# Last GEMM of a fused attention and two-MLP kernel: seven products for both halves of K in two of its three units

## The chip, the cores and the metric

The kernel runs on one core of a Trainium2 chip. The time is that of the device in microseconds. Before the change it is 571.29 us, the median of three runs (570.75 to 573.59).

## The reference, cut to what matters

```
attn  = softmax(30 * tanh(q k^T / 8 / 30)) v          # 2 batches, 12 heads, 448 positions, 64 wide
x     = attn as 896 tokens x 768
x     = leaky(x @ w_in) @ w_out                       # 768 -> 2048 -> 768, slope 0.01
xn    = x / rms(x) * rms_g
out   = (silu(xn @ w_gate) * (xn @ w_val)) @ w_out2   # 768 -> 1536 -> 768
```

All in float32. The last line's second product is "the last GEMM": K = 1536, 768 output rows (the features; everything is held transposed), 896 columns (tokens).

## The kernel before, in words

Activations lie as 128 features by 448 tokens (S = 448), one such tile for each batch b, weights as 128 by 384 slabs (HALF). A float32 matrix is split into a high part (rounded to fp32r) and a low part (the rest), and a product is three matmuls: high weight by high activation, high by low, low by high. K is taken in 128-row steps (index c), three in a half of 384.

**Seven products.** A block of two row tiles by two batches is computed from seven half-size products instead of eight (Strassen's form as Winograd wrote it). P1, P5, P7, P6, P3, P2, P4 take, in this order, the activation operands B11, T1, T3, T2, B22, B21, T4. T1 to T4 are sums or differences of activation tiles; the weights of P5, P7, P6, P3 are sums too (`s_sum`, made by DVE in `s_part`). Each product is 9 matmuls (3 steps of K, 3 matmuls each). Its results are put together on DVE (`take_p5`, `take_p7`, `take_p6`, then the `value`, `gate` or `result` functions), and ACT keeps P1 in SBUF (`keep_p1`).

**Units.** The program counts units s. 8 to 19 are the twelve units of gate and value (seven products each, K = 768 whole), 20, 21, 22 the three units of the last GEMM (`UNITS` = 20, `LAST` = 23). In this text they are G12 for unit 19 and L1, L2, L3 for the last three. G12 makes the last two of 24 activation tiles (`weighted_1`, `weighted_0`, into `act_full`). In each of L1, L2, L3 the kernel before takes the first half of K (tiles 0 to 5) plainly, as eight half-size products (`plain`; weights PA, PB, PC, PD, 72 matmuls), and the second half (tiles 6 to 11) by the seven products (63 matmuls): 135 matmuls a unit. The operands are made once, before and in L1: plain splits by ACT and POOL during units 11 to 19, T1 to T4 and their splits around the joint of G12 and L1.

**Order.** It is written out by hand, engine by engine; every engine runs its list in order and waits on semaphores. A weight slab n goes through ACT (`weight_hi`: copy to the high part, once product n - 7 has freed the slot in a ring of seven), then POOL (`weight_lo`: raw less high), then PE. For four of seven the raw operand is an `s_sum` slot, which DVE may only rewrite when POOL has made the low part of the slab before in that slot. Raw weights come by DMA on SP's queue into four buffers, each loaded when POOL is done with the one before it there. Names and lines of before that the argument touches: `weight_hi` L648, `weight_lo` L538, `keep_p1` L656, `s_part` L972 to L981, `take_p5` L996, `take_p7` L1002, `take_p6` L1008, `z_t3` L1253, `z_t2` L1258, `z_t4` L1263, `z_lo` L1267, `z_hi` L835, the results L1274 to L1298, `product` L1509, `plain` L1686.

Of the kernel before, what the change touches and what calls it, by code (L numbers as in the profile page):

```python
# [17 lines left out]
def build(nc, qk, v, cap, w_in, w_out, w_gate, w_val, w_out2, rms_g, out, recips):  # L18
# [67 lines left out]

    with ExitStack() as ctx:
# [284 lines left out]
        def plain_hi(k, b):  # L372
            i = PLAIN.index((k, b))
            return plain_ring[:, cols(i)] if i < 8 else plain_spare[:, cols(i - 8)]

        def plain_lo(k, b):
            return act_lo[:, cols(2 * k + b)]

        def z_tile(blk, c):
            return {B22: act_tile(F0 + KH + c, 1), B21: act_tile(F0 + KH + c, 0), T3: act_tile(F0 + c, 1)}.get(blk, act_tile(F0 + c, 0))

        def t1(k, c):
            return k[:, cols(c)]

        def z_parts(*blks):
            return [(blk, c) for blk in blks for c in range(KH)]

        z_all = z_parts(B11, T3, T2, B22, B21, T4)  # L390
        z_count = {part: i + 1 for i, part in enumerate(z_all)}
# [1372 lines left out]
```

## Time and profile before

| | |
|---|---|
| median of 3 runs | 571.29 us (570.75 to 573.59) |
| the profiled execution's own time | 573.29 us |
| its span in the trace | 571.5 us |
| PE busy | 565.1 us, 99% |
| DVE, ACT, POOL busy | 68%, 50%, 54% |
| granted TensorE clock | 0.999 of full |

The profile is of one execution, whose time is 1.8 us more than its span and 2.0 us more than the median. Busy shares are means over stages. A row of a timeline has the start in us from the span's start, the duration in us, engine, line, operation, output <- inputs, shapes, how many were merged, and in brackets the idle time before it and what ended it. A matmul row lasts 0.37 us, but the next starts 0.20 us after it.

### The profile page before, as it was taken

Reading aid. Unit: us, or ns where it says so; the run is one execution under the profiler, and the core shown is the slowest. Engines: PE = TensorE matmul, PEld = TensorE weight load, DVE = VectorE, ACT = ScalarE, POOL = GpSimd, SP = SyncE. Lnnn points to the kernel's source line nnn. Section 1 sums busy time; section 2 is a strip of 40 time slices with the busy share of each in tenths; the row PEclk is TensorE's granted clock in tenths of the full one; section 3 lists DMA queues with packets and bytes.
Section 4 is the critical chain, followed back from the end, with each engine's and each line's share of the span. In section 5 each row is a group of like instructions: output and inputs, shape, how many; then the busy total and the mean of one; then the engine's idle time right before and its main releaser. Section 6 shows DMA issues by size and latency. Waiting matters only on the chain.

```text
span 571.5 us, 7775 instructions
## 1 busy us (share of the span) xinstructions
PE 565.1 (99%) x2724; PEld 475.1 (83%) x2724; DVE 390.2 (68%) x543; ACT 287.1 (50%) x495; POOL 310.5 (54%) x269
## 2 busy tenths in 40 slices
PE   9999999999999999999999999999999999999997
PEld 5544554688999999999999989999999999989996
DVE  4479897695555454335975599988888989991513
ACT  6889888226444564345644456444444453631210
POOL 1035463569566553335652577777868785554440
PEclk9999999999999999999999999999999999999999
DMA  6355432213111141110210011122111111041401
GB/s 170 96 173 164 107 111 62 51 44 111 57 55 56 60 135 55 57 56 28 84 55 29 1 56 57 56 83 84 57 55 56 56 55 57 0 143 42 148 18 64
DMA packets 29717, 41.48 MB, mean 73 GB/s; under 512 B 17008, under 2 KB 18672, under 8 KB 29680
## 3 DMA queue, kind: packets, MB, share of 16 engines
q1 hardware_dynamic: 29536, 40.99, 23.2%
q8 instruction: 22, 0.36, 0.3%
q14 instruction: 15, 0.12, 0.1%
q10 hardware_dynamic: 144, 0.00, 0.0%
HBM read 38.15 MB, written 2.80 MB: 72 GB/s over the span
## 4 chain that ended last, share of the span: by engine, by line
PE 96%; DVE 2%; issue 1%; ACT 1%; ACTq 0%; DVEq 0%
PE ps L1509 51%; PE ps L1576 21%; PE ps L1432 9%; PE ps L1686 7%; PE ps L1420 4%; PE ps L1438 2%; PE ps L1424 1%; PE ps L1518 1%; DVE act_full L1263 1%; ACT x_hi L835 0%; DVE x_raw L911 0%; DVE x_lo L1267 0%; PE ps L1628 0%; DVE sums_eps L917 0%; PE ps L1651 0%
## 5 line engine op out<-in xcount | busy, mean ns | idle before, releaser
L538 POOL TENSOR_TENSOR w_lo<-w_raw,w_hi 128x384 fp32r<-128x384 f32 x113 | 132.8, 1180 | 157.7 <-ACT w_hi L648 157.2
L1509 PE MATMUL ps<-x_hi,w_hi 128*128 128x448 f32 x474 | 174.5, 368 | 0.0
L1509 PE MATMUL ps<-x_hi,w_lo 128*128 128x448 f32 x474 | 173.6, 366 | 0.0
L1509 PE MATMUL ps<-x_lo,w_hi 128*128 128x448 f32 x474 | 173.6, 366 | 0.0
L538 POOL TENSOR_TENSOR w_lo<-s_sum,w_hi 128x384 fp32r<-128x384 f32 x92 | 104.8, 1150 | 55.5 <-ACT w_hi L648 55.5
L1509 PEld LDWEIGHTS ps<-x_hi,w_hi 128*128 128x128 f32 x474 | 89.0, 188 | 9.3 <-issue 1.3
L1509 PEld LDWEIGHTS ps<-x_hi,w_lo 128*128 128x128 f32 x474 | 89.0, 188 | 7.8
L1509 PEld LDWEIGHTS ps<-x_lo,w_hi 128*128 128x128 f32 x474 | 89.0, 188 | 7.7
L648 ACT ACTIVATE w_hi<-s_sum 128x384 fp32r<-128x384 f32 x92 | 47.8, 523 | 91.5 <-PE ps L1509 69.5
L648 ACT ACTIVATE w_hi<-w_raw 128x384 fp32r<-128x384 f32 x113 | 57.7, 515 | 32.9 <-PE ps L1686 18.5
L1432 PE MATMUL ps<-probs,v_ones 128*65 128x448 f32 x144 | 56.6, 541 | 0.2 <-DVE x_raw L911 0.2
L624 ACT ACTIVATE probs<-ps,capc 128x896 f32<-128x896 f32 (+1 forms) x48 | 42.0, 901 | 12.3 <-PE ps L1420 11.0
L1432 PEld LDWEIGHTS ps<-probs,v_ones 128*65 128x65 f32 x144 | 19.3, 137 | 30.3 <-issue 29.1
L631 ACT ACTIVATE probs<-probs,capc 128x1344 f32<-128x1344 f32 (+2 forms) x25 | 41.1, 1644 | 0.8
L1086 DVE TENSOR_TENSOR x_lo<-g,x_hi 128x448 fp32r<-128x448 f32 x32 | 22.1, 736 | 23.5 <-ACT x_hi L682 23.5
L1086 DVE TENSOR_TENSOR ring_lo<-g,ring_hi 128x448 fp32r<-128x448 f32 x32 | 24.5, 811 | 15.2 <-ACT ring_hi L682 15.2
L682 ACT ACTIVATE ring_hi<-g 128x448 fp32r<-128x448 f32 x32 | 16.6, 569 | 22.5 <-PE ps L1576 22.5
L682 ACT ACTIVATE x_hi<-g 128x448 fp32r<-128x448 f32 x32 | 16.6, 570 | 21.8 <-PE ps L1576 21.8
L1576 PE MATMUL ps<-ring_hi,w_lo 128*128 128x448 f32 x96 | 27.5, 368 | 0.0
L1576 PE MATMUL ps<-ring_hi,w_hi 128*128 128x448 f32 x96 | 27.5, 367 | 0.0
L1576 PE MATMUL ps<-ring_lo,w_hi 128*128 128x448 f32 x96 | 27.5, 368 | 0.0
L1576 PE MATMUL ps<-x_lo,w_hi 128*128 128x448 f32 x96 | 27.3, 366 | 0.0
(162 smaller groups left out, 938.5 us busy)
## 6 DMA issues: line engine op xcount, KB each, us to landing
w_raw<-in_w_out SPq DMA_DIRECT2D x28, 384.0 KB, 3.3
w_raw<-in_w_in SPq DMA_DIRECT2D x16, 384.0 KB, 4.1
qk_raw<-in_qk SPq DMA_DIRECT2D x11, 480.0 KB, 4.2
w_raw<-in_w_gate SPq DMA_DIRECT2D x12, 384.0 KB, 3.1
w_raw<-in_w_val SPq DMA_DIRECT2D x12, 384.0 KB, 3.7
v_ones<-in_v SPq DMA_DIRECT2D x12, 224.0 KB, 3.3
recip_row<-recips SPq DMA_DIRECT2D x12, 224.0 KB, 3.5
out<-sq SPq DMA_DIRECT2D x6, 224.0 KB, 1.9
```

Of the source, the lines that this page charges most:

```text
L538: pool.tensor_tensor(w_lo[:, c], source, w_hi[:, c].bitcast(F32), ALU.subtract).then_inc(w_lo_done, 1)
L624: act.activation(tiles(probs_of(p, i, n), S), ps[:, bank_of(p, i):bank_of(p, i) + n, 0:S], ACT.Tanh, scale=capc[:, 4:5]).then_inc(tanh_don ...
L631: act.activation(c, c, ACT.Exp, scale=capc[:, 2:3], bias=capc[:, 6:7]).then_inc(exp_done, 1)
L648: act.activation(w_hi[:, c], w_source(n), ACT.Copy).then_inc(w_hi_done, 1)
L682: act.activation(ring(i, b, ring_hi, x_hi), g_tile(2 * f + b), ACT.Copy).then_inc(g_hi_done, 1)
L1086: dve.tensor_tensor(ring(i, b, ring_lo, x_lo), g_tile(2 * f + b), ring(i, b, ring_hi, x_hi).bitcast(F32), ALU.subtract).then_inc(g_lo_done, 1)
L1420: last = pe.matmul(ps[:, bank + h, 0:S], k[HEAD[h], k_c], q[HEAD[h], 0:S], start=(k is hi and q is hi), stop=(k is lo))
L1432: pe.matmul(ps[0:D + 1, pv_bank(p) + h, 0:S], v_ones[p % 2][:, c:c + D + 1], probs[p % 2][:, (2 * t + h) * S:(2 * t + h + 1) * S], start=( ...
L1438: last = pe.matmul(ps[0:D + 1, pv_bank(p) + h, 0:S], v_ones[p % 2][HEAD[h], c:c + D + 1], probs[p % 2][HEAD[h], 2 * MAIN * S:(2 * MAIN + 1 ...
L1509: last = pe.matmul(ps[:, base(s) + to, 0:S], w[:, w_c], x, start=(j in (P1, P5, P7, P6) and c == 0 and first), stop=(c == KH - 1 and w is ...
L1576: last = pe.matmul(ps[:, ROW_BANK[m] + b, 0:S], w[:, w_c], ring(i, b, beside, in_x), start=(f == 0 and w is w_hi and x == "hi"), stop=(f = ...
L1686: last = pe.matmul(ps[:, base(s) + to, 0:S], w[:, w_c], x(k, b), start=((row, b, k) == (0, 0, 0) and w is w_hi and x is plain_hi), stop=(k ...
```

## The change

L1 now computes the seven products of the first half of K (part 0) and takes the second half (part 1) plainly. L2 and L3 take both halves by seven products: first P1, P5, P7, P6 of part 0 and of part 1, then P3, P2, P4, each for part 0 and part 1 (in L3 P4 ahead of P2), the two parts summed in the same PSUM banks. So the operands of the seven products are needed for both parts: those of part 0 are made from unit 10 on (sums on DVE, splits of three of them on ACT and POOL), T2, B22, B21, T4 of part 0 and B11, B12 of part 1 at the joint and in L1, B21, B22 and all four T of part 1 in L1 and at its end. Each of L2 and L3 has two sets of weight sums. P1 is copied out of its own bank and stays in it, so a result in bank A needs one operation, not two. At the joint, DVE's gate operations stand ahead of splits.

The core of the diff (what is left out are the buffers, semaphores and counts that go with it):

```diff
-    LAST_ORDER = [P1, P5, PA, PB, P7, PC, P6, PD, P3, P2, P4]
+    LAST_ITEMS = [[(P1, 0), (P5, 0), (P7, 0), (P6, 0), (PA, 1), (PC, 1), (P3, 0), (P2, 0), (P4, 0), (PB, 1), (PD, 1)],
+                  [(j, part) for part in (0, 1) for j in (P1, P5, P7, P6)] + [(j, part) for j in (P3, P2, P4) for part in (0, 1)],
+                  [(j, part) for part in (0, 1) for j in (P1, P5, P7, P6)] + [(j, part) for j in (P3, P4, P2) for part in (0, 1)]]
...
+        EARLY_SPLITS = {U1 + 4: (0,), U1 + 5: (1,), U1 + 6: (2,), U1 + 8: (3, 4), U1 + 9: (5, 6), U1 + 10: (7, 8)}
+        EARLY_SUMS = {U1 + 2: [(T1, 0)], U1 + 3: [(T1, 1)], U1 + 4: [(T1, 2)], U1 + 5: [(T3, 0)], U1 + 6: [(T3, 1), (T2, 0)],
+                      U1 + 7: [(T3, 2), (T2, 1)], U1 + 8: [(T2, 2), (T4, 0)], U1 + 9: [(T4, 1)], U1 + 10: [(T4, 2)]}
...
@@ scalar: the order of L2
+            s = UNITS + 1
+            last_weights(s, (P1, 0))
+            z_upper(1, T1)
+            last_weights(s, (P5, 0), (P7, 0), (P6, 0), (P1, 1))
+            z_upper(1, T3)
+            last_weights(s, (P5, 1))
+            z_upper(1, T2)
+            last_weights(s, (P7, 1), (P6, 1))
+            z_upper(1, T4)
+            keep_p1(s)
+            last_weights(s, *LAST_ITEMS[1][8:])
...
@@ vector: a sum of part 1 takes the slot of part 0
+            def s_part(s, j, part=0):
+                r, made = raw_of(s) + 2 * part, sums_before(s, part)
+                if part == 1:
+                    dve.wait_ge(w_lo_done, widx(s, j) + 1)
...
+            def result_11(s):
+                dve.wait_ge(act_done, 2 * N2)
+                at_least(dve, out_sem[O11], 16 * (s - UNITS))
+                wait_result(s, P2, PB)
+                dve.tensor_tensor(sq[0][:, :], bank(s, BANK_A), r_bc[:, cols(0)], ALU.mult).then_inc(o11_done, 1)
...
@@ vector: the order from the joint to the start of L2's results
             take_p7(s)
-            z_lo(B11, 1)
-            z_lo(B11, 2)
             take_p6(s)
             value_22(s)
-            z_lo(T3, 0)
+            z_lo(1, B11, 0)
             gate_sum(s)
             gate_12(s)
-            z_lo(T3, 1)
+            z_lo(1, B11, 1)
+            z_lo(1, B11, 2)
+            gate_11(s)
             weighted_1(s)
-            z_t3(2)
-            gate_11(s)
-            take_p5(s + 1)
-            s_part(s + 1, P6)
-            z_lo(T3, 2)
+            z_lower(0, T2)
             value_21(s)
             weighted_0(s)
...
             s = UNITS
+            take_p5(s)
+            z_lo(1, B12, 0)
             take_p7(s)
+            z_lo(1, B12, 1)
+            z_lo(1, B12, 2)
             take_p6(s)
+            z_lower(0, B22)
+            z_lower(0, B21)
+            z_lower(0, T4)
+            z_lower(1, B21)
+            z_lower(1, B22)
+            s_parts(s + 1)
+            z_sums(T1)
+            z_lower(1, T1)
+            s_part(s + 1, P5, 1)
+            z_sums(T3)
+            z_sums(T2)
+            result_11(s)
+            result_12(s)
+            s_part(s + 1, P7, 1)
+            z_lower(1, T3)
+            result_21(s)
             result_22(s)
+            z_sums(T4)
+            z_lower(1, T2)
+            s = UNITS + 1
+            s_part(s, P6, 1)
+            s_part(s, P3, 1)
+            z_lower(1, T4)
+            take_p5(s)
+            take_p7(s)
+            take_p6(s)
...
@@ tensor: what L2 and L3 wait for
+            def last_product(s, j, part):
+                n = widx(s, j, part)
+                pe.wait_ge(w_lo_done, n + 1)
+                if part == 0:
+                    bank_free(s, j)
+                for c in range(KH):
+                    if (s, part) == (UNITS, 0) and j in (B11, T1, T3):
+                        pe.wait_ge(early_lo_done, early_count[j, c])
+                    elif (s, part) in ((UNITS, 0), (UNITS + 1, 1)):
+                        pe.wait_ge(z_lo_done, z_count[part, j, c])
...
+            for j in (P1, P5, P7, P6):
+                last_product(UNITS, j, 0)
+            plain_half(0)
+            for j in (P3, P2, P4):
+                last_product(UNITS, j, 0)
+            plain_half(1)
+            for s in range(UNITS + 1, LAST):
+                for j, part in LAST_ITEMS[s - UNITS]:
+                    last_product(s, j, part)
```

DVE's list of before, from the end of L1's first result to L2's `take_p5` (the last row). `u` and `a_t` are the half-made results, `sq` the others, `r_bc` the scale, `s_sum` the weight sums:

```order
L1276 TENSOR_TENSOR a_t_60<-a_t_60,r_bc 128x448 [waits c22_done]
L972 TENSOR_TENSOR s_sum<-w_raw_52 128x384 [waits raw_in1,w_lo_done]
L975 TENSOR_TENSOR s_sum<-w_raw_51,w_raw_52 128x384 [waits raw_in0,w_lo_done]
L978 TENSOR_TENSOR s_sum<-s_sum,w_raw_51 128x384 [waits s_done,w_lo_done]
L981 TENSOR_TENSOR s_sum<-w_raw_51,s_sum 128x384 [waits s_done,w_lo_done]
L1283 TENSOR_TENSOR sq_68<-ps,u_0_62 128x448 [waits prod_done,act_done,u2_done]
L1285 TENSOR_TENSOR sq_68<-sq_68,r_bc 128x448 [waits c12_done]
L1290 TENSOR_TENSOR sq_67<-ps,p_0_58 128x448 [waits prod_done]
L1292 TENSOR_TENSOR sq_67<-sq_67,r_bc 128x448 [waits c11_done]
L1296 TENSOR_TENSOR u_0_62<-ps,u_0_62 128x448 [waits prod_done]
L1298 TENSOR_TENSOR u_0_62<-u_0_62,r_bc 128x448 [waits c21_done]
L996 TENSOR_TENSOR a_t_61<-ps,p_1_59 128x448 [waits prod_done,p1_kept]
```

The same engine in the changed program, the last twelve rows up to L2's `take_p5`. L1021, L1024 and L1027 are the sums of part 1 for P7, P6 and P3; L1321 is a low part, L1312 the T4 sums:

```order
L1021 TENSOR_TENSOR s_sum<-w_raw_53,w_raw_54 128x384 [waits raw_in2,w_lo_done]
L1321 TENSOR_TENSOR act_lo<-act_full,act_lo 128x448 [waits t2_done1,z_hi_done] x3
L1357 TENSOR_TENSOR u_0_62<-ps,u_0_62 128x448 [waits prod_done]
L1359 TENSOR_TENSOR u_0_62<-u_0_62,r_bc 128x448 [waits c21_done]
L1364 TENSOR_TENSOR a_t_60<-ps,a_t_60 128x448 [waits prod_done,a2_done]
L1366 TENSOR_TENSOR a_t_60<-a_t_60,r_bc 128x448 [waits c22_done]
L1312 TENSOR_TENSOR act_full<-act_full 128x448 [waits z_lo_done,t2_done1,act_done] x3
L1321 TENSOR_TENSOR act_lo<-act_full,x_hi 128x448 [waits t4_done1,z_hi_done] x3
L1024 TENSOR_TENSOR s_sum<-s_sum,w_raw_53 128x384 [waits s_done,w_lo_done]
L1027 TENSOR_TENSOR s_sum<-w_raw_53,s_sum 128x384 [waits s_done,w_lo_done]
L1321 TENSOR_TENSOR act_lo<-act_full,x_lo 128x448 [waits z_hi_done] x3
L1042 TENSOR_TENSOR a_t_61<-ps,p_1_59 128x448 [waits prod_done,p1_kept]
```

The results of L1 and the sums for P6 and P3 of part 1 now stand behind the sums and splits of part 1's operands. ACT's list of before, from the last operand split to `keep_p1` of L2 (L656) and one slab more:

```order
L835 ACTIVATE x_hi<-act_full 128x448 [waits t4_done,prod_done] x3
L648 ACTIVATE w_hi<-w_raw_51 128x384 [waits raw_in0,prod_done]
L648 ACTIVATE w_hi<-s_sum 128x384 [waits s_done,prod_done]
L648 ACTIVATE w_hi<-w_raw_53 128x384 [waits raw_in2,prod_done] x2
L648 ACTIVATE w_hi<-s_sum 128x384 [waits s_done,prod_done]
L648 ACTIVATE w_hi<-w_raw_54 128x384 [waits raw_in3,prod_done]
L648 ACTIVATE w_hi<-s_sum 128x384 [waits s_done,prod_done]
L648 ACTIVATE w_hi<-w_raw_54 128x384 [waits raw_in3,prod_done]
L656 ACTIVATE p_1_59<-ps 128x448 [waits u2_done,prod_done]
L648 ACTIVATE w_hi<-s_sum 128x384 [waits s_done,prod_done]
```

And in the changed program, from L2's first slab to the two slabs of P3 (L685 is `weight_hi`, L873 `z_hi`, L691 `keep_p1`):

```order
L685 ACTIVATE w_hi<-w_raw_51 128x384 [waits raw_in0,prod_done]
L873 ACTIVATE x_lo<-x_lo_f_101 128x448 [waits t1_done1,prod_done] x3
L685 ACTIVATE w_hi<-s_sum 128x384 [waits s_done,prod_done] x3
L685 ACTIVATE w_hi<-w_raw_53 128x384 [waits raw_in2,prod_done]
L873 ACTIVATE act_lo<-act_full 128x448 [waits z_lo_done,t3_done1,prod_done] x3
L685 ACTIVATE w_hi<-s_sum 128x384 [waits s_done,prod_done]
L873 ACTIVATE x_hi<-act_full 128x448 [waits t2_done1,prod_done] x3
L685 ACTIVATE w_hi<-s_sum 128x384 [waits s_done,prod_done] x2
L873 ACTIVATE x_lo<-act_full 128x448 [waits t4_done1,prod_done] x3
L691 ACTIVATE p_1_59<-ps 128x448 [waits u2_done,prod_done]
L685 ACTIVATE w_hi<-s_sum 128x384 [waits s_done,prod_done] x2
```

Four groups of operand splits now stand between the weight slabs of L2, and both slabs of P3 behind `keep_p1`.

## Rows read from the trace of the kernel before

**Rows 1.** The page, part 1: busy us, share of the span, instructions.
```profile
PE 565.1 (99%) x2724; PEld 475.1 (83%) x2724; DVE 390.2 (68%) x543; ACT 287.1 (50%) x495; POOL 310.5 (54%) x269
```
**Rows 2.** What PE waited for: us in total, times, longest.
```profile
PE ps L1686 <- DVE u L1008: 1.3, 1, 1.3
```
**Rows 3.** The chain that ended last: start us, us, what.
```profile
496.51 1.97 DVE x_lo L1267 x2
498.48 4.07 DVE act_full L1263 x3
502.55 0.55 DVE u L1008
...
529.12 5.54 PE ps L1686 x27
534.66 9.15 PE ps L1509 x45
...
567.75 0.64 DVE u L1296
568.41 0.62 DVE u L1298
```
**Rows 4.** Timeline of PE: L1's first matmul, the stall, L2's first, the last.
```profile
483.29 0.36 PE L1509 MATMUL ps<-x_hi,w_hi 128*128 128x448 f32 x1
...
503.14 0.47 PE L1686 MATMUL ps<-plain_ring,w_hi 128*128 128x448 f32 x1 [1.30 <-DVE u L1008]
...
512.40 0.37 PE L1509 MATMUL ps<-x_hi,w_hi 128*128 128x448 f32 x1
...
567.35 0.36 PE L1509 MATMUL ps<-x_hi,w_lo 128*128 128x448 f32 x1
```
**Rows 5.** Timeline of DVE around the joint, single instructions and runs.
```profile
471.80 1.44 DVE L1236 TENSOR_TENSOR act_full<-u,sq 128x448 f32<-128x448 f32 x1
473.16 0.61 DVE L1244 TENSOR_TENSOR t_tile<-act_full 128x448 f32<-128x448 f32 x1
...
498.40 4.15 DVE L1263 TENSOR_TENSOR act_full<-act_full 128x448 f32<-128x448 f32 x3
502.47 0.61 DVE L1008 TENSOR_TENSOR u<-ps,p 128x448 f32<-128x448 f32 x1
503.01 3.29 DVE L1267 TENSOR_TENSOR x_lo<-act_full,x_hi 128x448 fp32r<-128x448 f32 x6
507.21 0.63 DVE L1274 TENSOR_TENSOR a_t<-ps,a_t 128x448 f32<-128x448 f32 x1 [0.91 <-PE ps L1686]
507.87 0.63 DVE L1276 TENSOR_TENSOR a_t<-a_t,r_bc 128x448 f32<-128x448 f32 x1
508.41 0.55 DVE L972 TENSOR_TENSOR s_sum<-w_raw 128x384 f32<-128x384 f32 x1
508.88 0.55 DVE L975 TENSOR_TENSOR s_sum<-w_raw,w_raw 128x384 f32<-128x384 f32 x1
```
**Rows 6.** Timeline of POOL: low parts of weights, beside a busy and an idle DVE.
```profile
499.31 2.75 POOL L538 TENSOR_TENSOR w_lo<-w_raw,w_hi 128x384 fp32r<-128x384 f32 x2
...
509.66 1.11 POOL L538 TENSOR_TENSOR w_lo<-s_sum,w_hi 128x384 fp32r<-128x384 f32 x1 [2.49 <-ACT w_hi L648]
...
518.04 1.02 POOL L538 TENSOR_TENSOR w_lo<-s_sum,w_hi 128x384 fp32r<-128x384 f32 x1
```
**Rows 7.** Timeline of ACT: a run of splits, a weight slab, `keep_p1`.
```profile
494.54 2.90 ACT L835 ACTIVATE x_hi<-act_full 128x448 fp32r<-128x448 f32 x6
...
509.06 0.53 ACT L648 ACTIVATE w_hi<-s_sum 128x384 fp32r<-128x384 f32 x1 [3.19 <-DVE s_sum L972]
...
514.86 0.53 ACT L656 ACTIVATE p<-ps 128x448 f32<-128x448 f32 x1
```
**Rows 8.** DMA issues from 440 us on: median us to landing.
```profile
w_raw<-in_w_out SPq DMA_DIRECT2D x12, 384.0 KB, 4.1
```
**Rows 9.** Timeline of SP: the last store.
```profile
569.06 0.33 SPq L514 DMA_DIRECT2D out<-u  x1
```

More of the change, by code:

```diff
@@ L41, in build @@
     P1, P5, P7, P6, P3, P2, P4, PA, PB, PC, PD = range(11)
-    B11, T1, T3, T2, B22, B21, T4 = range(7)
+    B11, T1, T3, T2, B22, B21, T4, B12 = range(8)
     BANK_A, BANK_B, BANK_C, BANK_D = range(4)
@@ L376, in plain_lo @@
[L376 to L391, printed above, removed]
+        B_TILE = {B11: (0, 0), B12: (0, 1), T3: (0, 1), B21: (KH, 0), B22: (KH, 1)}
@@ new lines, in build, with z_place @@
+        B_TILE_1 = {B11: (0, 0), T2: (0, 0), B12: (0, 1), T3: (0, 1), B21: (KH, 0), T4: (KH, 0), B22: (KH, 1)}
+        SUM_TILE = {T1: 24, T2: 27, T4: 30}
+        def z_place(part, blk, c, whole, acc, x):
+            if part == 0:
+                if blk in B_TILE:
+                    k, b = B_TILE[blk]
+                    return whole[:, cols(2 * (k + c) + b)]
+                return acc if (blk, c) == (T4, 2) else whole[:, cols(SUM_TILE[blk] + c)]
+            if blk == T1:
+                return x[:, xs(T2, c)]
+            k, b = B_TILE_1[blk]
+            return whole[:, cols(2 * (2 * KH + k + c) + b)]
@@ new lines, in build @@
+        EARLY_SUMS = {U1 + 2: [(T1, 0)], U1 + 3: [(T1, 1)], U1 + 4: [(T1, 2)], U1 + 5: [(T3, 0)], U1 + 6: [(T3, 1), (T2, 0)],
+                      U1 + 7: [(T3, 2), (T2, 1)], U1 + 8: [(T2, 2), (T4, 0)], U1 + 9: [(T4, 1)], U1 + 10: [(T4, 2)]}
+        Z = [(part, blk, c) for part, blk in ((1, B11), (0, T2), (1, B12), (0, B22), (0, B21), (0, T4), (1, B21), (1, B22),
+                                              (1, T1), (1, T3), (1, T2), (1, T4)) for c in range(KH)]
+        z_count = {part: i + 1 for i, part in enumerate(Z)}
@@ L887, in _ @@
-            z_upper(B21)
-            last_weights(s, P3, P2, P4)
-            z_upper(T4)
-            for s in range(UNITS + 1, LAST):
-                last_weights(s, P1, P5, PA, PB, P7, PC, P6, PD)
-                keep_p1(s)
-                last_weights(s, P3, P2, P4)
+            last_weights(s, (P1, 0))
+            z_upper(1, B11)
+            last_weights(s, (P5, 0), (P7, 0))
+            z_upper(0, T2)
+            z_upper(1, B12)
+            last_weights(s, (P6, 0))
+            silu(s - 1, 1)
@@ L1401, in _ @@
+            s_part(s, P6, 1)
+            s_part(s, P3, 1)
+            take_p5(s)
+            take_p7(s)
+            take_p6(s)
+            result_22(s)
+            result_12(s)
+            result_21(s)
+            result_11(s)
         @block.tensor
@@ L1504, in product @@
                     w_c = slice(n % 7 * HALF + c * 128, n % 7 * HALF + (c + 1) * 128)
-                    high, low = x_hi[:, xs(j, c)], x_lo[:, xs(j, c)]
-                    if s >= UNITS and j == P5:
-                        high, low = t1_hi[c][:, :], t1(t1_lo, c)
-                    for w, x, first in ((w_hi, high, True), (w_hi, low, False), (w_lo, high, False)):
-                        last = pe.matmul(ps[:, base(s) + to, 0:S], w[:, w_c], x,
-                                         start=(j in (P1, P5, P7, P6) and c == 0 and first),
+                    for w, x in ((w_hi, x_hi), (w_hi, x_lo), (w_lo, x_hi)):
+                        last = pe.matmul(ps[:, base(s) + BANK_OF[j], 0:S], w[:, w_c], x[:, xs(j, c)],
+                                         start=(j in (P1, P5, P7, P6) and c == 0 and w is w_hi and x is x_hi),
                                          stop=(c == KH - 1 and w is w_lo), skip_group_check=(j in (P3, P2, P4)))
@@ L1679, in plain @@
[L1679 removed]
+                    pe.wait_ge(((p1_kept, a_done), (a2_done, u2_done))[row][b], s + 1)
+                to, blk = ((BANK_A, BANK_C), (BANK_D, BANK_B))[row][b], ((B11, B12), (B21, B22))[half][b]
                 for c in range(KH):
[L1681 to L1683 removed]
+                    pe.wait_ge(z_lo_done, z_count[1, blk, c])
```

451 lines of the change are left out of this document (214 added, 237 removed).

## The prediction

> **What bounds the kernel now.** I read the page's busy shares first, then what PE waited for, then the chain that ended last, then the timelines of PE, DVE, POOL and ACT around the joint of G12 and L1. PE is busy 99% of the span [rows 1], so the time is the number of matmuls by their pitch, plus the few places where PE stands. In the last GEMM it stands once, 1.3 us, for L1's `take_p6` [rows 2]. The chain shows what had made DVE late there: before 502.55 us it runs through low parts and T4 sums on DVE, behind it through PE alone to the tail [rows 3]. So DVE is the second engine that counts, at the joint only. Two prices follow from the chain: 27 plain matmuls take 5.54 us (0.205 each), 45 from x_hi and x_lo 9.15 (0.203) [rows 3].
>
> **What it takes away.**
> 1. Matmuls. L2 and L3 have 14 products of 9, 126 matmuls, where 135 were: 18 fewer. L2 starts at 512.40 and the last matmul at 567.35, 0.2 before its slot ends [rows 4], so a unit takes 27.6. Of the 126, 54 read an operand outside x_hi and x_lo (part 0 of B11, T1, T3; the low parts of other T, B22, B21; all of part 1's T3), which I price as the plain ones, 72 as the others: 11.1 + 14.6 = 25.7. Two units save 3.7 us.
> 2. The stall. L1 runs from 483.29 to 512.40 [rows 4], 29.1 us for 135 slots worth 27.5. In the changed list `take_p6` of L1 stands ahead of the splits of B22, B21 and T4, and comes (below) 3 to 4 us before PE needs it. L1 then ends at 510.8: 1.6 us saved.
> 3. The tail. The last product was P4, with two DVE operations behind it (0.64 and 0.62) [rows 3], then the store [rows 9]. Now it is P2, with one: 0.65 us saved. The stores before it are done earlier, so nothing new stands in front of it.
> Together 6.0 us. What PE does in units 8 to 19 is as before.
>
> For item 1 the Trainium skill has another price: by "TensorE: Matmul & The Clock Gate", section "Wait — 56ns, not 53.3ns?", a warm matmul takes its columns by 2.4 GHz and 2.5 ns, which would be 189 ns here and 3.4 us for 18. The rows show 203 to 205 at a granted clock of 0.999, and the rows decide.
>
> **What it adds: DVE at the joint.** More comes onto DVE between G12 and L2's P3 than before: part 1's T sums and splits can't be made before G12's last tiles, and L2 wants them for its products of part 1. The prices, as start-to-start: an operation with one input in PSUM 0.54 (502.47 to 503.01), one with both inputs in SBUF 0.535 (six in 3.29, the last 0.61 long: 2.68 by five), a weight sum 0.47 (508.41 to 508.88) [rows 5]. Beside a POOL instruction the second kind takes 1.36 (471.80 to 473.16) or 1.37 (three in 4.07) [rows 3, 5], the PSUM kind no more than alone; POOL's own goes from 1.02 to 1.38 [rows 6]. So each POOL instruction that meets SBUF work costs DVE 0.83.
> - From 473.16 to L1's `take_p6` DVE has 27 operations, 14.4 us, and nine weight slabs beside them. Ten of the 27 read PSUM, and waits are few; followed one by one the slabs cost 0.55 each, 4.9 together. DVE is through at 492.5. PE's own P6 allows 490.9 + 0.5 at the earliest.
> - From there to the sum for P6 of part 1 there are 49: 15 low parts (B22, B21, T4 of part 0, B21, B22 of part 1), four sums of L2, T1 and its low parts (6), the sum for P5 of part 1, T3 and T2 (6), three operations of results, the sum for P7, T3's low parts (3), four of results, T4 and T2's low parts (6). 43 x 0.535 + 6 x 0.47, and 0.5 for pairs that wait on each other: 26.3. Nine slabs fall into it (PB, PD of L1; P1, P5, P7, P6 and P1, P5, P7 of part 1 of L2). One meets an operation that reads PSUM, eight cost 0.83, and 0.2 is waited for P5's slab: 6.9. So the sum for P6 of part 1 starts at 492.5 + 26.3 + 6.9 = 525.7. Call it X.
>
> The Trainium skill's "SBUF — State Buffer", section "Who interferes with whom", says that a DVE instruction with two SBUF inputs blocks fully against a GpSimd one that reads SBUF, for the whole instruction. The rows show the block, yet 0.83 per slab and not the whole 1.02. By the whole, nine slabs would cost 9.2, and X would be 528.0.
>
> **What waits for it.** From the sum's start to PE: 0.65 until ACT starts (508.41 to 509.06), 0.60 until POOL starts (to 509.66), 1.0 and 0.1 [rows 5 to 7]: 2.35. PE wants P6 of part 1 seven products after L2's start, 510.8 + 7 x 1.84 = 523.7. It gets it at 528.0: 4.3 late. And a second wait follows. DVE's next row is the sum for P3 of part 1, which may overwrite its slot only when POOL has done P3 of part 0. That slab stands on ACT behind P6's, three splits of T4 (1.45, half of the run of six) and `keep_p1` (a slab or `keep_p1` 0.53, of which the next overlaps some 0.1, as in that run) [rows 7]: ACT starts it at X + 0.65 + 0.45 + 1.45 + 0.45 = X + 3.0, and its low part is done 1.6 later, at X + 4.6. Behind the waiting sum stand three low parts of T4 and `take_p5`, which frees the bank that PE's P3 goes to. The sum 0.5, three low parts 1.6, one slab beside them 0.83, `take_p5` 0.6: X + 7.4 to X + 8.2, 533.5. PE wanted P3 at 525.5. So L2 is 8.0 us late in all (P6's 4.3 are in it).
>
> Other new waits I cost at nothing. L1: the low parts of B22 are done at 496.2 and wanted at 498.0; B21, T4 and part 1's B21, B22 keep 1 to 2 us. L3's raw weights: issued at X + 7.7 to X + 10 as L2's P2 and P4 slabs are done, 4.1 to land [rows 8], P5's slab ready by X + 16.2; PE wants it at X + 20.7. L3's P3: `take_p5` is 2 us early. The early sums in units 10 to 18 add one or two DVE operations a unit where PE does not wait for DVE at all [rows 2]. SP: L3's loads stand behind four stores of L1 that are ready before. If the cover in L1 is gone, it costs what DVE is then late, up to 1 or 2 us.
>
> **The sum.** -6.0 + 8.0 = +2.0 us. Against the profiled execution, span 571.5 to 573.5 and its time 573.3 to 575.3; that execution was 2.0 above the median, so on the median 571.3 + 2.0 = 573.3 us.
>
> Bounds of X. From below: DVE at PE's heels, 491.4, and no slab in its way: 491.4 + 26.3 = 517.7. Then P3 waits for nothing: -6.0, 565.3. From above: `take_p6` at 494 and nine slabs by their whole 1.02: 494 + 26.3 + 9.2 = 529.5, P3 at 537.3, 11.8 late: +5.8, 577.1. I take 525.7, since DVE's rows of the same stretch (three in 4.07 beside POOL, six in 3.29 without) show both prices; one us of X is one us of the time.
>
> **The rivals.**
> - Faster. DVE keeps up: POOL's slabs fall beside PSUM work or DVE's turns come first, and P6's sum is made by 518. For it: POOL has gaps there (2.49 before its slab at 509.66) [rows 6], and a slab that falls beside a PSUM read is free. Against it: 49 operations without a gap, 45 of them on SBUF alone. 565.3. A half-way case (X at 521 to 523) gives 568.5 to 570.5, since P3's wait comes before P6's.
> - Clearly slower. DVE's list is late already in L1: the splits of B22 or T4 come after PE's P3 or P4. They have 1 to 2 us of cover; two more slabs in DVE's way (1.7) and a late `weighted_0` (1 to 2) use it up, and then PE stands in L1 and again in L2, for X moves with it. It decides from `take_p6` 2 us later than 492.5. X of 528 to 529.5: 575.6 to 577.1. The skill's whole-instruction block belongs here, with 528.0 and 575.6.
> - The change doesn't do what it says: the diff's lists hold 14 products of 9 for L2 and L3 each, so this is out.
>
> **How the numbers follow.** The forecast as worked out (X 523.5 to 527.5: 571.1 to 575.1) 0.50; full cover 0.20; half-way 0.12; clearly slower 0.18. Under about 0.5%, 2.9 us, a measurement of this kernel can't tell from no change. Slower by more (over 574.2): a third of the forecast's chance and nearly all of the slow case, 0.34. Faster by more (under 568.4): full cover and a little of the half-way, 0.23. Within: 0.43. The range leaves out the ends of both: 566.5 to 577.0; the likeliest case alone 571.1 to 575.1.
>
> **What would show it.** PE's list of waits: two new entries in L2, at `last_product`, one for POOL's `w_lo` of about 4 us near 524 to 528, one for DVE's `a_t` (`take_p5`) of 3 to 4 us near 530 to 534. L2 starting at 510.8; P6's sum on DVE at 525.7; DVE with no idle from 473 to 530 but in front of P3's sum, where it waits for POOL some 4 us. L3 of 25.7 us without a wait. One DVE operation behind the last matmul. Wrong would be: no such waits (the cover held), PE standing in L1 (the backlog is larger), or L3 longer than 25.8 (its pitch or its loads).

## The result, and the profile after

The changed kernel is slower. It was timed twice, each time beside runs of the kernel before:

| | changed | before | ratio (95% interval) |
|---|---|---|---|
| first, 4 runs | 578.65 us | 572.44 us | 1.0108 (1.0059 to 1.0157) |
| again, 6 runs | 576.95 us | 572.25 us | 1.0080 (1.0056 to 1.0104) |

The second is the tighter one: 4.6 us slower (3.2 to 6.0), where 2.0 was forecast. Before itself came out 1 us higher than in the three runs that the prediction went by (572.3 for 571.3). The forecast of 573.3 is 3.7 below 576.95; 1.0 of this is the reference and 2.6 the change's own effect. Of the two medians the first lies above the end of the stated range, 577.0, and the second 0.05 below it.

Part 1 of the page of the changed kernel (busy us, share of the span, instructions), against [rows 1]:

```profile
PE 562.9 (98%) x2706; PEld 473.6 (82%) x2706; DVE 411.9 (72%) x575; ACT 294.1 (51%) x513; POOL 313.0 (54%) x272
```

The 18 matmuls are gone (2706 for 2724), DVE has 32 operations more. The page's row of granted clock, in forty slices, says what its shares don't:

```profile
PEclk9999999999999999999999999999999999998899
```

Two slices show an 8; in before that row is forty nines. What PE waited for in the last GEMM, where before had the one entry of [rows 2] (us in total, times, longest):

```profile
PE ps L1741 <- POOL w_lo L575: 4.7, 1, 4.7
PE ps L1741 <- DVE a_t L1042: 2.1, 1, 2.1
```

These are the two entries that the prediction named, one for POOL's weights (forecast some 4 us) and one for `take_p5` (forecast 3 to 4 us). PE's timeline has their places, the first matmuls of L2 and L3 and the last one, against [rows 4]:

```profile
510.29 0.37 PE L1741 MATMUL ps<-z_ring,w_hi 128*128 128x448 f32 x1
...
523.03 0.37 PE L1741 MATMUL ps<-act_lo,w_lo 128*128 128x448 f32 x1
528.08 0.74 PE L1741 MATMUL ps<-x_hi,w_hi 128*128 128x448 f32 x1 [4.68 <-POOL w_lo L575]
...
530.86 0.57 PE L1741 MATMUL ps<-act_lo,w_hi 128*128 128x448 f32 x1
531.23 0.57 PE L1741 MATMUL ps<-x_hi,w_lo 128*128 128x448 f32 x1
533.94 0.71 PE L1741 MATMUL ps<-x_hi,w_hi 128*128 128x448 f32 x1 [2.14 <-DVE a_t L1042]
...
535.20 0.58 PE L1741 MATMUL ps<-x_hi,w_hi 128*128 128x448 f32 x1
535.57 0.58 PE L1741 MATMUL ps<-act_lo,w_hi 128*128 128x448 f32 x1
...
537.40 0.36 PE L1741 MATMUL ps<-x_hi,w_hi 128*128 128x448 f32 x1
537.60 0.37 PE L1741 MATMUL ps<-x_lo,w_hi 128*128 128x448 f32 x1
...
546.57 0.37 PE L1741 MATMUL ps<-z_ring,w_hi 128*128 128x448 f32 x1
...
572.21 0.37 PE L1741 MATMUL ps<-x_hi,w_lo 128*128 128x448 f32 x1
```

The reader is to see two things. PE stands at 523.23 for 4.85 us and at 531.60 for 2.34 us. And between 528.08 and 537.40 the matmuls last some 0.57 and follow each other at 0.37 (530.86 to 531.23, 535.20 to 535.57), where all others last 0.37 and follow at 0.20 (537.40 to 537.60). The table of stretches gives the reason. Its columns are PE's busy us and matmuls, the granted clock, the DMA share and GB/s:

```profile
482.00:511.00 29.00, 29.00 (x144) 1.00 0.18 55
511.00:528.00 17.00, 12.40 (x61) 0.97 0.15 54
528.00:538.00 10.00, 7.79 (x21) 0.53 0.22 58
538.00:576.00 38.00, 34.58 (x169) 0.99 0.21 76
```

and the third stretch of the kernel before:

```profile
528.00:538.00 10.00, 10.00 (x51) 1.00 0.52 180
```

In 528 to 538 the granted clock is 0.53, that is the lower of the two levels (1.2 GHz) nearly throughout, after PE had stood. It is back at the upper one at 537.40.

The units, from first matmul to first matmul:

| us | L1 | L2 | L3, to its last matmul's start | from there to the end |
|---|---|---|---|---|
| before | 29.11 | 27.58 | 27.37 | 4.15 |
| changed | 27.62 | 36.28 | 25.64 | 3.49 |
| change | -1.49 | +8.70 | -1.73 | -0.66 |

The sum is +4.8. The profiled spans differ by 4.2 (575.7 for 571.5), since L1 begins at 482.67 in this execution and at 483.29 in that of before. In the other profiles it begins between 481.24 (e6) and 482.87 (e3), so the end of the front part scatters by more than that from one execution to the next. Before's is the latest of the ten profiles; whether the change has a part in that isn't shown.

### The profile page after: what moved, and what is told of

Read it like the earlier page. It is cut to its first block, busy times and chain, and to the rows that moved or that the text cites. A ratio compares the mean times of both kernels' runs of the same rounds, so it can differ in the third digit from the quotient of the medians.

```text
span 575.7 us, 7855 instructions
## 1 busy us (share of the span) xinstructions
PE 562.9 (98%) x2706; PEld 473.6 (82%) x2706; DVE 411.9 (72%) x575; ACT 294.1 (51%) x513; POOL 313.0 (54%) x272
## 4 chain that ended last, share of the span: by engine, by line
PE 90%; DVE 4%; DMA 2%; issue 1%; ACT 1%; POOL 1%; SPq 0%; DVEq 0%; ACTq 0%
PE ps L1577 43%; PE ps L1644 20%; PE ps L1741 10%; PE ps L1512 9%; PE ps L1500 3%; PE ps L1758 3%; PE ps L1518 2%; DMA qk_raw<-in_qk 1%; PE ps L1504 1%; DVE act_lo L1321 1%; DVE x_raw L955 1%; DMA sums<-x_raw 1%; POOL x_lo L586 0%; DVE s_sum L1024 0%; ACT probs L668 0%
## 5 line engine op out<-in xcount | busy, mean ns | idle before, releaser
L575 POOL TENSOR_TENSOR w_lo<-s_sum,w_hi 128x384 fp32r<-128x384 f32 x100 | 113.4, 1146 | 77.7 <-ACT w_hi L685 77.6
L1577 PE MATMUL ps<-x_hi,w_hi 128*128 128x448 f32 x420 | 154.2, 367 | 0.1
L1577 PE MATMUL ps<-x_hi,w_lo 128*128 128x448 f32 x420 | 153.4, 365 | 0.0
L1577 PE MATMUL ps<-x_lo,w_hi 128*128 128x448 f32 x420 | 153.4, 365 | 0.0
L685 ACT ACTIVATE w_hi<-s_sum 128x384 fp32r<-128x384 f32 x100 | 51.5, 523 | 98.4 <-PE ps L1577 52.7
L1577 PEld LDWEIGHTS ps<-x_hi,w_hi 128*128 128x128 f32 x420 | 78.9, 188 | 7.9 <-issue 1.0
L1577 PEld LDWEIGHTS ps<-x_hi,w_lo 128*128 128x128 f32 x420 | 78.9, 188 | 6.3
L1577 PEld LDWEIGHTS ps<-x_lo,w_hi 128*128 128x128 f32 x420 | 78.9, 188 | 6.2
L685 ACT ACTIVATE w_hi<-w_raw 128x384 fp32r<-128x384 f32 x111 | 56.3, 514 | 13.4 <-PE ps L1577 7.0
L1027 DVE TENSOR_TENSOR s_sum<-w_raw,s_sum 128x384 f32<-128x384 f32 x25 | 27.1, 1082 | 14.4 <-POOL w_lo L575 12.2
L1741 PE MATMUL ps<-act_lo,w_hi 128*128 128x448 f32 x84 | 31.2, 382 | 0.0
L1018 DVE TENSOR_TENSOR s_sum<-w_raw 128x384 f32<-128x384 f32 x25 | 22.8, 914 | 7.4 <-DMA w_raw<-in_w_in 6.5
```

What stands on the lines that cost most here:

```text
L575: pool.tensor_tensor(w_lo[:, c], source, w_hi[:, c].bitcast(F32), ALU.subtract).then_inc(w_lo_done, 1)
L685: act.activation(w_hi[:, c], w_source(n), ACT.Copy).then_inc(w_hi_done, 1)
L1018: dve.tensor_tensor(dst, m2[:, lower], m2[:, upper], ALU.add).then_inc(s_done, 1)
L1027: dve.tensor_tensor(dst, m1[:, upper], s_sum[:, cols(2, HALF)], ALU.subtract).then_inc(s_done, 1)
L1577: last = pe.matmul(ps[:, base(s) + BANK_OF[j], 0:S], w[:, w_c], x[:, xs(j, c)], start=(j in (P1, P5, P7, P6) and c == 0 and w is w_hi and ...
L1741: last = pe.matmul(ps[:, base(s) + BANK_OF[j], 0:S], w[:, w_c], x(part, j, c), start=(j in (P1, P5, P7, P6) and part == 0 and c == 0 and w ...
```

## The experiments

There are seven kernels and one repetition. e1 to e4 stand beside runs of before at 572.72 us, the repetition, e5 and e6 beside runs at 572.25, e7 beside runs at 572.89.

**e1: the results of L1 later.** On DVE the seven operations of L1's four results go behind `take_p6` of L2.

```diff
             z_sums(T2)
-            result_11(s)
-            result_12(s)
             s_part(s + 1, P7, 1)
             z_lower(1, T3)
-            result_21(s)
-            result_22(s)
             z_sums(T4)
...
             take_p6(s)
+            result_11(s - 1)
+            result_12(s - 1)
+            result_21(s - 1)
+            result_22(s - 1)
             result_22(s)
```

> The changed kernel with one move on DVE: the seven operations of L1's four results (4.1 us) stand behind take_p6 of L2 instead of ahead of the sum for P6 of part 1. Theory (DVE's queue is what L2 waits for): that sum starts 4.0 us earlier, at about 521.7 instead of 525.77, P6 of part 1 waits about 0.8 us instead of 4.85, P3 still waits for take_p5 (sum + 8.2 = 529.9) and is 4.1 us earlier than 533.94; behind it the lower clock costs up to 1.6 as now. Together -4.1 us against the changed kernel (-5.7 if the clock then stays up). Rival (the weight slabs on ACT and POOL bound P6 of part 1, not DVE's order): the first PE wait stays near 4.8 and the time within 1 us of the changed kernel.

Measured: 574.41 us, ratio 1.0032 (1.0016 to 1.0049), which is 2.7 us less than the changed kernel by the ratios (1.0080 less 1.0032), not 4.1. DVE's timeline, one weight sum on the way, the sum for P6 of part 1 and `take_p5`:

```profile
515.39 1.37 DVE L1021 TENSOR_TENSOR s_sum<-w_raw,w_raw 128x384 f32<-128x384 f32 x1
...
522.33 0.54 DVE L1024 TENSOR_TENSOR s_sum<-s_sum,w_raw 128x384 f32<-128x384 f32 x1
...
529.75 0.61 DVE L1042 TENSOR_TENSOR a_t<-ps,p 128x448 f32<-128x448 f32 x1
```

And PE's, with the two waits and two matmuls of the slow stretch:

```profile
524.62 0.47 PE L1741 MATMUL ps<-x_hi,w_hi 128*128 128x448 f32 x1 [1.39 <-POOL w_lo L575]
524.93 0.36 PE L1741 MATMUL ps<-act_lo,w_hi 128*128 128x448 f32 x1
...
530.50 0.71 PE L1741 MATMUL ps<-x_hi,w_hi 128*128 128x448 f32 x1 [3.77 <-DVE a_t L1042]
...
532.13 0.57 PE L1741 MATMUL ps<-act_lo,w_hi 128*128 128x448 f32 x1
532.51 0.57 PE L1741 MATMUL ps<-x_hi,w_lo 128*128 128x448 f32 x1
```

DVE's queue is what sets X (the start of that sum), and both waits move with it. X at 522.33 is 3.4 earlier, 3.3 of it against L1's start. It isn't the 4.1 of the seven operations, since a slab of POOL that ran beside two reads of PSUM in the changed kernel (515.19 there) now meets the weight sum at 515.39, which takes 1.37 us for 0.55. P3 stands 20.38 us behind L2's start, where it was 23.65. Of these 3.3 only 2.2 arrive at the end of L2, which takes 34.11 for 36.28. The clock has the rest. The first stand, 1.6 us, leaves P6 of part 1 at 0.20 a matmul; the second, 3.9 us, drops the clock, and the 15 matmuls from 530.50 to 535.87 take 5.74 where 3.1 is usual. That is 2.7 too much behind P3's start; the changed kernel pays 1.6 there.

The 2.7 is that of the profiled execution. The 12 runs of e1 fall into two kinds by their mean granted clock: 0.994 to 0.996 (8 runs, mean 574.9 us, the profiled one among them) and 0.997 (4 runs, 573.4 us). e2 has the same two: 0.994 (7 runs, 574.8) and 0.997 (5 runs, 573.5). So the stretch at the lower level is shorter in some executions, and those take some 1.4 us less. In the repetition of the changed kernel the runs at 0.990 and at 0.994 have the same mean (576.95), but they are only 2 and 4.

**e2: the bank before the sum.** Behind the sum for P6 of part 1, `take_p5` and `take_p7` come first, and ACT does `keep_p1` and P3 of part 0 ahead of T4's splits.

```diff
             s_part(s, P6, 1)
-            s_part(s, P3, 1)
-            z_lower(1, T4)
             take_p5(s)
             take_p7(s)
+            s_part(s, P3, 1)
+            z_lower(1, T4)
             take_p6(s)
...
-            z_upper(1, T4)
             keep_p1(s)
-            last_weights(s, *LAST_ITEMS[1][8:])
+            last_weights(s, (P3, 0))
+            z_upper(1, T4)
+            last_weights(s, *LAST_ITEMS[1][9:])
```

> The changed kernel with the order behind the sum for P6 of part 1 turned: take_p5 and take_p7 of L2 on DVE ahead of the P3 sum of part 1 and T4's low parts, and keep_p1 and the slab of P3 of part 0 on ACT ahead of T4's splits. Theory (the second wait is DVE standing behind POOL with take_p5 queued behind it): the sum for P6 stays at 525.8 and the first PE wait at 4.8, the second wait (2.34) goes, so -2.3 us; if the clock comes back as early as the work is without a break, another -0.5 to -1.6. Rival (P3 is bound by its own slab or by T4's operands): a second wait of 2 us or more stays and the time is that of the changed kernel within 1 us.

Measured: 574.36 us, ratio 1.0039 (1.0020 to 1.0057), 2.3 less than the changed kernel. The second wait is gone from the list and the first is unchanged, 4.7. PE's timeline:

```profile
528.05 0.74 PE L1742 MATMUL ps<-x_hi,w_hi 128*128 128x448 f32 x1 [4.68 <-POOL w_lo L575]
...
533.80 0.37 PE L1742 MATMUL ps<-x_hi,w_hi 128*128 128x448 f32 x1
534.01 0.36 PE L1742 MATMUL ps<-act_lo,w_hi 128*128 128x448 f32 x1
```

L2 takes 33.37, 2.9 less. The slow matmuls are 15, not 18, and 6 of them stand behind P3's start, not 9. So the second wait was made by the order alone: in the changed kernel DVE stood 4 us in front of the P3 sum with `take_p5` queued behind it. The edit turns the order on DVE and on ACT, and no run separates the two.

**e3: both moves**, and the sum for P6 of part 1 directly behind that for P7.

```diff
             s_part(s + 1, P7, 1)
+            s_part(s + 1, P6, 1)
             z_lower(1, T3)
```

> Both moves, and the sum for P6 of part 1 directly behind that for P7 of part 1. Theory (order alone makes L2 late; the work fits): no PE wait over 0.5 us in L2, the granted clock stays at its upper level, L2 takes 25.8 to 26.3 instead of 36.28, so -10 us against the changed kernel, about 568 to 569, and 4 us below the kernel before. Rival (the capacity of DVE, ACT and POOL at the joint is short whatever the order): the waits move to P3 or P2 of part 1 and over 3 us of them stay, so -7 or less. A third: the stall moves to L3, whose sums now stand behind L1's results.

Measured: 570.91 us, ratio 0.9969 (0.9953 to 0.9985). It is faster than before by 1.8 us, where 4 were expected. L2 takes 28.73, no row has a clock under the upper level, and of PE's waits in L2 and L3 four short ones are left:

```profile
523.97 0.44 PE L1742 MATMUL ps<-x_hi,w_hi 128*128 128x448 f32 x1 [0.36 <-DVE act_lo L1322]
...
528.53 0.47 PE L1742 MATMUL ps<-x_hi,w_hi 128*128 128x448 f32 x1 [0.66 <-POOL w_lo L575]
...
539.23 0.47 PE L1742 MATMUL ps<-z_ring,w_hi 128*128 128x448 f32 x1 [1.26 <-POOL w_lo L575]
...
541.72 0.48 PE L1742 MATMUL ps<-z_ring,w_hi 128*128 128x448 f32 x1 [0.38 <-POOL w_lo L575]
```

The two last are the first two products of L3 (z_ring holds B11 and T1 of part 0), so a part of the gain was turned into a new wait, at L3. SP's timeline has the likely cause, which e6 and e7 test:

```profile
532.68 0.33 SPq L551 DMA_DIRECT2D out<-u  x1
534.04 0.33 SPq L551 DMA_DIRECT2D out<-a_t  x1
534.41 1.89 SPq L511 DMA_DIRECT2D w_raw<-in_w_out  x4
```

The four loads of L3 stand behind all stores of L1's results, which e3 makes late on DVE. POOL had made the low part that frees the first buffer by 529.8, over 4 us before.

**e4: PE kept busy.** The changed kernel with throw-away matmuls in front of the two waits. Their results go to a bank that nothing reads.

```diff
+            def filler(n):
+                pe.wait_ge(o11_done, 1)
+                x = z_high(1, B22, 0)
+                for _ in range(n):
+                    pe.matmul(ps[:, base(UNITS) + BANK_A, 0:S], x[:, 0:128], x, start=True, stop=True)
...
                 for j, part in LAST_ITEMS[s - UNITS]:
+                    if (s, j, part) == (UNITS + 1, P6, 1):
+                        filler(20)
+                    if (s, j, part) == (UNITS + 1, P3, 0):
+                        filler(16)
```

> The changed kernel with throw-away matmuls on PE in front of its two waits of L2: 20 before P6 of part 1 (4 us) and 16 before P3 (3.2 us), into L1's free bank A, from a tile that is there; no other engine's list changes. Theory (behind the two waits PE runs at its lower clock because it stood): P6 of part 1 starts at 528.1 as now, its nine matmuls take 1.84 instead of 3.5, P3 starts at 533.9 as now, its nine matmuls take 1.84 instead of 3.46, the granted clock of 528 to 538 is near 1 instead of 0.53, and L3 starts 1.6 us earlier: -1.6 us in all. Rival (those matmuls are slow because of contention for SBUF or PSUM with DVE, ACT and POOL at that place): the pitch stays at 0.37 and the time does not fall.

Measured: 575.9 us, ratio 1.0067 (1.0050 to 1.0084): 0.7 below the changed kernel by the ratios, each of them uncertain by more than that. The trace is clearer. PE's timeline, with the throw-away matmuls at L1778:

```profile
527.57 0.47 PE L1741 MATMUL ps<-x_hi,w_hi 128*128 128x448 f32 x1 [0.62 <-POOL w_lo L575]
527.87 0.37 PE L1741 MATMUL ps<-act_lo,w_hi 128*128 128x448 f32 x1
...
529.51 3.46 PE L1778 MATMUL ps<-x_hi 128*128 128x448 f32 x16
533.45 0.44 PE L1741 MATMUL ps<-x_hi,w_hi 128*128 128x448 f32 x1 [0.48 <-DVE a_t L1042]
```

Behind both waits the matmuls follow at 0.20 again from the second on (in the nine of P3 too). The stretch of 528 to 538 has a clock of 1.00 for 0.53:

```profile
528.00:538.00 10.00, 9.52 (x47) 1.00 0.24 89
```

L2 began at 509.78 here, and both products stand as late in it as in the changed kernel (P6 at +17.79, P3 at +23.67; there +17.79 and +23.65). Only what follows P3 is shorter: L2 takes 34.79, 1.5 less than 36.28. DVE, ACT and POOL do the same beside it, so contention isn't what slowed those matmuls. The lower clock is, and it follows PE's standing.

**The changed kernel again.**

> The changed kernel once more, unchanged, on the chip and beside the same runs of before as the two below: its first comparison gave 1.0108 with an interval of plus or minus 0.005. From the trace the difference is +4.2 of span, of which -0.6 is scatter of the front part: +4.8 us, a ratio of 1.0084. If the first ratio holds it is 6.2 us.

Measured: 576.95 us, ratio 1.0080 (1.0056 to 1.0104), as the trace had it (1.0084) and not as the first ratio. In its profile L2 takes 36.13 us and has the same two waits (4.7, 2.1).

**e5: before, with `take_p6` earlier.** The second term of the prediction by itself.

```diff
+            take_p6(s)
             for c in range(KH):
                 z_t4(c)
-            take_p6(s)
```

> The kernel before with take_p6 of L1 ahead of the three T4 sums on DVE, nothing else. Theory of the prediction's second term (PE's only wait in the last GEMM is that, and removing it is worth 1.3 to 1.6 us): the wait of 1.3 is gone, L1 lasts 27.6 instead of 29.1, -1.5 us against before. Rival (T4's splits, 1.9 us later now, become late for P4, or PE's 1.6 of excess has another cause): under 0.5 us.

Measured: 570.58 us, ratio 0.9967 (0.9952 to 0.9983), 1.9 us below before (1.0 to 2.7). PE's list of waits has nothing behind 470 us any more. From L1's first plain matmul to the last matmul of all it takes 78.84 us (486.19 to 565.03) where before took 80.39 (486.96 to 567.35): 1.55 less. DVE's row of it, where that of before is the 502.47 of [rows 5]:

```profile
499.27 0.62 DVE L1008 TENSOR_TENSOR u<-ps,p 128x448 f32<-128x448 f32 x1 [1.53 <-PE ps L1509]
```

DVE now waits for PE there, no longer PE for DVE.

**e6: order and loads.** e3 and three things more, for what e3 had left.

```diff
-            store(UNITS)
-            load_last(UNITS + 2)
+            store(UNITS, RESULTS[0][:2])
+            load_last(UNITS + 2, (0, 1))
+            store(UNITS, RESULTS[0][2:3])
+            load_last(UNITS + 2, (2, 3))
+            store(UNITS, RESULTS[0][3:])
+            sp.wait_ge(out_sem[O22], 16)
...
-            z_sums(T4)
-            z_lower(1, T2)
+            for c in range(KH):
+                z_sum(1, T4, c)
+                z_lo(1, T2, c)
             s = UNITS + 1
             take_p5(s)
+            s_part(s, P3, 1)
             take_p7(s)
-            s_part(s, P3, 1)
...
             result_22(s)
-            result_12(s)
             s_parts(s + 1)
+            result_12(s)
```

> The earlier order with both moves, and three things more for what was left of waits in it (0.5 and 0.8 us in L2, 1.3 and 0.5 in L3): T4's sums and T2's low parts of part 1 in turn and the P3 sum of part 1 ahead of take_p7; L3's first two loads on SP's queue ahead of L1's last two stores; L3's weight sums on DVE ahead of one of L2's results. Theory (what the change takes away is the 5.7 us that the trace shows, and the rest of the waits is order): no PE wait over 0.4 us behind 482, L2 and L3 25.8 each, 5.7 us below before, ratio 0.990. Rival (L3's loads can't land in time, since their buffers come free only with L2's P2 and P4 slabs): 1 to 2 us of waits stay at L3's P5 and the ratio is 0.993 to 0.996.

Measured: 568.26 us, ratio 0.9932 (0.9911 to 0.9953): 3.9 us below before (2.7 to 5.1), 8.5 below the changed kernel by the ratios. The rival's size came true, not 5.7. SP's wait for `out_sem[O22]` in the diff holds L2's stores until L1's last one has landed. PE's timeline has two waits in L2 and one at L3's first product, where PE stands 0.9 us (0.3 more at the second):

```profile
523.72 0.47 PE L1747 MATMUL ps<-x_hi,w_hi 128*128 128x448 f32 x1 [0.39 <-DVE act_lo L1326]
...
526.65 0.47 PE L1747 MATMUL ps<-x_hi,w_hi 128*128 128x448 f32 x1 [0.24 <-POOL w_lo L579]
...
536.87 0.47 PE L1747 MATMUL ps<-z_ring,w_hi 128*128 128x448 f32 x1 [0.74 <-POOL w_lo L579]
```

L3's first slab had to wait for its raw weights, whose load was issued only behind L1's second store, at 531.20:

```profile
535.22 0.53 ACT L689 ACTIVATE w_hi<-w_raw 128x384 fp32r<-128x384 f32 x1 [8.28 <-DMA w_raw<-in_w_out]
```

**e7: loads first.** e6, with each of L3's loads ahead of one of the stores.

```diff
-            store(UNITS, RESULTS[0][:2])
-            load_last(UNITS + 2, (0, 1))
-            store(UNITS, RESULTS[0][2:3])
-            load_last(UNITS + 2, (2, 3))
-            store(UNITS, RESULTS[0][3:])
+            for k in range(4):
+                load_last(UNITS + 2, (k,))
+                store(UNITS, RESULTS[0][k:k + 1])
```

> The kernel e6 with each of L3's four loads ahead of one of L1's four stores on SP's queue, the first load ahead of all. In e6 L3's first slab came at 535.2 and its first products lost 0.9 and 0.3 us. Theory (the loads stood behind the stores, not behind their buffers: POOL had freed the first at 527.9, and its load was issued at 531.2): the first load is issued at 528, L3's first slab is ready by 534, the waits at L3's P1 and P5 go, L2 28.0 becomes 27.0 and the time is 1.3 us under e6, ratio 0.991. Rival (the buffers or the transfer itself, 3.5 to 4 us, decide): L3's first wait stays at 0.7 and the ratio at 0.993.

Measured: 567.79 us, ratio 0.9922 (0.9904 to 0.9940): 4.5 us below before (3.4 to 5.5), the fastest of all here, though its interval and e6's overlap. The trace is clearer. The first load is issued at 528.71, L3's first slab starts 3.3 earlier (4.0 against L1's start), so it was the stores ahead of the loads, and not the buffers as e6's rival had it. L3's wait is gone, and PE's list of waits in the last GEMM has two entries left, both in L2. ACT's row of that slab:

```profile
531.92 0.53 ACT L687 ACTIVATE w_hi<-w_raw 128x384 fp32r<-128x384 f32 x1 [4.26 <-DMA w_raw<-in_w_out]
```

L2 takes 27.03 and L3 25.65, where 25.8 (25.6 to the last matmul's start) is what a unit takes without any wait. From L1's start to the last matmul it is 80.31 us (481.98 to 562.29), 3.75 less than before's 84.06; 0.65 comes at the tail. So 4.4 of the 5.7 us that the change takes away are there, and 1.2 of the rest are the two waits.

## Why the prediction was wrong

The sign, the chain of waits and their places were right. What failed is the price of the slow side: the time in which PE stands was 0.9 us too small, and the lower clock behind it, 1.6 us, was not there at all.

- **Matmuls, -3.7.** Right: L3 has 126 in 25.84 us (25.64 and one slot), forecast 25.7, and L2 without a wait would be as long. Against before that is 3.5.
- **The stall of L1, -1.6.** Right: L1 took 27.62 us, 1.49 less, and e5 gets the same 1.55 from the kernel before alone. DVE's `take_p6` started at 492.13 and was through at 492.66, when the next operation started (forecast 492.5).
- **The tail, -0.65.** Right, 0.66.
- **X, the start of the sum for P6.** It started at 525.77, forecast 525.7, and that this agrees to 0.1 is luck. X goes with L1's start: it lies 43.1 us behind it in this profile, in the repetition, in e2 and in e4, whatever the execution, where the forecast has 42.4 (525.7 less 483.29). L1 merely began 0.6 earlier here. The 0.7 came in ahead of the work that the prediction counted. POOL has a new operand split at the joint, the weight slab behind it comes later, and it now meets `act_full` on DVE, where before it met a read of PSUM. The row of before, then those of the changed kernel:

```profile
471.27 0.61 DVE L1230 TENSOR_TENSOR act_full<-a_t,sq 128x448 f32<-128x448 f32 x1
```

```profile
468.85 1.55 POOL L643 TENSOR_TENSOR act_lo<-act_full,z_extra 128x448 fp32r<-128x448 f32 x1
470.64 1.34 DVE L1276 TENSOR_TENSOR act_full<-a_t,sq 128x448 f32<-128x448 f32 x1
...
492.13 0.61 DVE L1054 TENSOR_TENSOR u<-ps,p 128x448 f32<-128x448 f32 x1
...
493.73 1.44 DVE L1321 TENSOR_TENSOR act_lo<-act_full,x_hi 128x448 fp32r<-128x448 f32 x1
...
509.43 1.35 DVE L1018 TENSOR_TENSOR s_sum<-w_raw 128x384 f32<-128x384 f32 x1 [0.92 <-POOL w_lo L575]
...
525.77 0.55 DVE L1024 TENSOR_TENSOR s_sum<-s_sum,w_raw 128x384 f32<-128x384 f32 x1
530.29 0.56 DVE L1027 TENSOR_TENSOR s_sum<-w_raw,s_sum 128x384 f32<-128x384 f32 x1 [3.97 <-POOL w_lo L575]
...
533.19 0.61 DVE L1042 TENSOR_TENSOR a_t<-ps,p 128x448 f32<-128x448 f32 x1
```

  The 49 operations behind `take_p6` took 33.1 us, forecast 33.2. The price of 0.83 for a slab of POOL beside DVE's work on SBUF alone held (0.81 to 0.83, seven times). But seven slabs cost it, not eight, and DVE stood 0.92 for P5's slab where 0.2 was allowed: two errors that cancel. The block for the whole instruction, which the prediction takes from the Trainium skill's "SBUF — State Buffer", section "Who interferes with whom", would be 1.02 a slab, and with that this trace doesn't agree.
- **What waits for it, +8.0.** The chain was the right one, down to DVE's wait for POOL of "some 4 us" (3.97) in front of P3's sum. P3 started at 533.94, forecast 533.5. PE came to L2 at 510.29 and wanted P3 at 525.1, so it was 8.9 late, and the term 0.9 too small. Of this 0.7 is X against L1, 0.4 the way from X to P3 (8.2 us for 7.8), and 0.2 goes off again, since L1 and the eight products ahead took that much longer than forecast.
- **The step that failed: every matmul behind a wait was taken at the same pitch.** The sum held only the time in which PE stood. It stood for 4.85 us, and from then on ran at the lower clock. In P6 of part 1 this costs nothing, because the wait for `take_p5` behind it takes it in (1.7 us: 3.5 from 528.08 to 531.60, where 1.85 is usual; that wait was 2.1 for that reason, and not 3 to 4 as forecast). Behind P3 nothing does, and nine matmuls take 3.46 instead of 1.84: 1.6 us. That term was in no case and no rival. e4 takes it away and leaves both products where they were, and L2 is 1.5 shorter; in e1 it is 2.7, and the saving falls short by the difference.

Together (from the profiled executions): -5.7 instead of -6.0, and 8.9 + 1.6 = 10.5 instead of 8.0, which is +4.8 for +2.0. The rest of the miss against 576.95 is the median of before, 1.0 higher in later runs. Why the first median was 1.7 higher still stays open; its interval and the second one overlap.

As to the rivals, full cover and the half-way case fell, since X was not earlier than forecast. The clearly slower case came near the size (575.6 to 577.1) by the wrong mechanism: it had PE stand in L1, and L1 had no wait. Its bound is also why the range ended too low: 577.0 was built from the latest X alone, with no price for what the clock does after a wait.

In the changed kernel PE stood for POOL's weights, and the granted clock behind it was 0.53. That PE falls back to its lower clock when it has waited for a transfer is told in the Trainium skill, "TensorE: Matmul & The Clock Gate", section "HAM oscillation — how this bites in real kernels"; the trace agrees, with another engine in the place of the transfer. The page's section "Back-to-back issue gap" gives N by 1.2 GHz for the pitch at that level, 373 ns here, and the trace agrees (0.37). The prediction used that page for the price of a warm matmul and not for this.

## What to carry to other kernels

A wait of PE is to be priced at its length and at the lower clock behind it, where the next wait doesn't take that in; here 1.6 to 2.7 us in the profiled executions, behind stands of 3.9 to 4.9 us, some 1.4 less in others of the same kernel (e1, e2), and nothing behind one of 1.6 us. When an operation is put behind a wait on an in-order engine, look at what stands behind it that another engine needs: `take_p5` behind P3's sum, with `keep_p1` behind T4's splits on ACT, cost 2.3 us that another order gave back (e2). And when results are moved later to clear a queue, their stores move too, and with them the loads that are queued behind the stores (e3; e7 gives it back). Last, when two numbers of a forecast and a trace agree, compare them against the same event: X agreed from the span's start and was 0.7 off from L1's.

## What the runs showed of the hardware

The lower clock came behind PE's standing, and throw-away matmuls in its place kept the clock at 1.00 (e4), with DVE, ACT and POOL at the same work. The lower clock lasted 15 matmuls in the profiled e1 and e2, behind stands of 3.9 and 4.9 us with none after it, and for all 18 of P6 and P3 in the changed kernel, where a second stand of 2.3 us lay between. The first matmul behind even a short wait costs some 0.1 us of its own: in e1 the second follows it at 0.31 (524.62 to 524.93), not 0.20, at the full clock.

A slab of POOL beside an operation of DVE with both inputs in SBUF cost DVE 0.81 to 0.83 us; beside reads of PSUM it cost nothing. The slab at 515.19 shows both: in the changed kernel it ran beside two results read from PSUM (0.61 and 0.60 us), in e1 beside a weight sum (1.37 us for 0.55).
